# Attention output and x kept by channel: diagonal term on TensorE, three scans a round, later products turned, flag counted in round 4

## The chip, the cores and the metric

The kernel runs on one core of a Trainium2 chip. The core has TensorE (PE, matmuls; PEld is its weight load), VectorE (DVE), ScalarE (ACT), GpSimd (POOL) and SyncE (SP, which here issues the DMAs), each with its own instruction stream, joined by semaphores. The metric is the device time in microseconds; smaller is better. The kernel before has a median of 393.24 us over 3 runs (393.06 to 395.09). "Columns" below are the elements of a matmul's moving operand in the free dimension. An f32 matmul is recorded as two records (two passes); a matmul of operands marked fp32r is one record.

## The reference, cut to what matters

Three stages follow each other on a batch of 2, 768 tokens and 384 channels (8 heads of 48).

```python
# 1 attention with a decaying state, per head
for t in range(S):
    cur = einsum('bhd,bhe->bhde', u[None] * kt, vt)          # the diagonal term: only token t itself
    y[:, :, t] = einsum('bhd,bhde->bhe', rt, state + cur)
    state = wt[:, :, :, None] * state + einsum('bhd,bhe->bhde', kt, vt)
x = y by (batch, token, head*48)
# 2 gated block
h = gelu(x @ w_in);  u, v = halves of h (512 each);  v_n = (v - mean)/sqrt(var + 1e-6) * g_ln
v_s = einsum('ts,bsd->btd', w_sg, v_n) + b_sg;        x = x + (u * v_s) @ w_out
# 3 mixer
h = relu(x.T @ w_tok1) @ w_tok2;  u = x + h.T;        out = u + relu(u @ w_ch1) @ w_ch2
```

## The kernel before, in words

**Attention** runs in 12 chunks ("rounds") of 128 tokens, six per batch; chunk n is round n. The 8 heads lie in 4 pairs; a pair takes 112 partitions (48, 16 unused, 48). With w inside the chunk turned into running products, backward (`suf`, L886) and forward (`pre`, L897), k and r are scaled (`kp`, `rp`), so that one round is made of these products on TensorE: the scores kp x rp (`scores`, L1132), k turned to tokens by channels (`turn_kp`, L1140), the new state (`state_products`, L1159), and the output (`outputs`: the carried state times rp, L1178, plus the masked scores times v, L1182). The output has tokens on the partitions. The diagonal term r*u*k summed over a head's channels is made beside it: GpSimd multiplies r by k (L560) and by u (L568), VectorE sums over 48 channels (L919), GpSimd multiplies by v (L595), VectorE adds it to the output (L947).

The order on each engine is written out by hand. VectorE, in a round: two masks of the scores (L926), forward scans of the next chunk (a reciprocal and 4 scans of 127), the diagonal's sum, the output's sum, backward scans two chunks ahead (4 scans of 128), the state (L939). GpSimd: scale k of chunk n+1 (L578), r*k*u, scale r of chunk n+1 (L587), diagonal times v. In rounds 0 to 4 TensorE has a few matmuls on the identity as filler (L1272).

**A flag.** The scaling only holds for w in a range. ScalarE counts violations in ten pieces (`check_range`, L750, L752), TensorE sums them over the partitions (L1189), VectorE reduces the sum (`count_range`, L960 to L964), GpSimd loads it into a register, branches, and writes `flag` (L662). Work on x and on the later weights' low parts waits for the flag.

**The later products** have f32 accuracy by splitting each operand into a high part (fp32r) and the rest: every product is three matmuls (`three`, L1113 to L1115). High parts are copied by ScalarE (weights L820) or GpSimd, low parts are subtracted by GpSimd (weights L549) or VectorE. Weights pass through three landing buffers (`raw`). x lies by token; it is turned to channels by TensorE transposes before the first product of each stage ("xT", "uT", L1218). Jobs are named by kind, batch and index: v and u are the halves of x @ w_in, sg the token product, out, tok1, tok2, ch1, ch2. `SLOT` puts the first jobs between the parts of rounds 5 to 11 (three slots a round), `TAIL` lists the rest. A sg job is 18 matmuls of 384 columns, a u job 9 of 384, a v job 9 of 512.

Of the kernel before, what the change touches and what calls it, by code (L numbers as in the profile page):

```python
# [17 lines left out]
C = H * D  # L18
# [19 lines left out]
WR, KR, VR = 2, 2, 3  # L38
YR = 5
BR = 3  # L40
# [14 lines left out]
PIECES = ([("w_in", 2), ("w_in", 3), ("w_in", 0), ("w_in", 1)] + [("w_sg", i) for i in range(6)]  # L55
# [15 lines left out]
}  # L71
TAIL = ([("sg", 0, i) for i in range(3, 8)] + [("xT", 1, i) for i in range(6)] + [("out", 0, i) for i in range(6)]
        + [("v", 1, i) for i in range(6)] + [("u", 1, i) for i in range(8)] + [("sg", 1, i) for i in range(8)]
        + [("tok1", 0, i) for i in range(2)] + [("out", 1, i) for i in range(6)] + [("tok2", 0, i) for i in range(6)]
        + [("tok1", 1, i) for i in range(2)] + [("uT", 0, i) for i in range(6)] + [("tok2", 1, i) for i in range(6)]
        + [("ch1", 0, i) for i in range(NCF)] + [("uT", 1, i) for i in range(6)] + [("ch2", 0, i) for i in range(BT)]
        + [("ch1", 1, i) for i in range(NCF)] + [("ch2", 1, i) for i in range(BT)]
        + [("ch1", 2, i) for i in range(NCF)] + [("ch2", 2, i) for i in range(BT)])
# [3 lines left out]
OUT_BY = {"xT": "AD", "v": "A", "u": "A", "sg": "D", "out": "D", "tok1": "AD", "tok2": "D",  # L82
          "uT": "AD", "ch1": "AD", "ch2": "D"}
# [30 lines left out]
def build(nc, r, k, v, w, u, w_in, g_ln, w_sg, b_sg, w_out, tok1, tok2, ch1, ch2, w_turned, kr_turned, kr_rows, v_rows,  # L114
# [3 lines left out]
    y_slow = nc.dram_tensor("y_slow", (B * H, S, D), F32, kind="Internal").ap()  # L118
# [16 lines left out]
    x = at("x", XN, [PART, B, NC, C])  # L135
# [7 lines left out]
    wz = at("wz", Z + NC * FH, [PART, NC, NP, PART])  # L143
# [19 lines left out]
    wn = put("wn", [PART, WR, NP, PART])  # L163
    kr = put("kr", [PART, KR, 2, C])
    suf = put("suf", [PART, 2, NP, PART + 1])
    vn = put("vn", [PART, VR, C])
    pre = put("pre", [PART, NP, PART])
    kp = put("kp", [PART, NP, PART])
# [5 lines left out]
    yt = put("yt", [PART, BR, C])  # L174
    ub = put("ub", [PART, C])
    cmask = put("cmask", [PART, PART])
    ones = put("ones", [PART, PART])
    dg = put("dg", [PART, 2, H])
# [20 lines left out]
    krT = put("krT", [PART, KR, 2, NP, PART])  # L199
    u_row = at("u_row", Z + NC * FH - C, [1, C])  # L200
    rku = put("rku", [PART, 2, C])
# [5 lines left out]
    gy = put("gy", [PART, STEP, EW])  # L207
# [7 lines left out]
    with ExitStack() as ctx:  # L215
# [3 lines left out]
        def sem(name):  # L219
            return ctx.enter_context(nc.semaphore(name))  # L220

        w_in_, kr_in, krT_in, v_in = ([sem(f"{n}_in{i}") for i in range(ring)]
                                      for n, ring in (("w", WR), ("kr", KR), ("krT", KR), ("v", VR)))
# [3 lines left out]
        ub_in, gln_in, bsg_in = sem("ub_in"), sem("gln_in"), sem("bsg_in")  # L227
        ident_made, u_in, u_spread = sem("ident_made"), sem("u_in"), sem("u_spread")
# [7 lines left out]
        rp_done, rk_done, rku_done, base_done, flagged = (sem("rp_done"), sem("rk_done"), sem("rku_done"),  # L236
                                                          sem("base_done"), sem("flagged"))
# [8 lines left out]
        w_hi, w_hi_act, w_split, x1_hi, x1_split, stored = (sem("w_hi"), sem("w_hi_act"), sem("w_split"), sem("x1_hi"), sem("x1_split"),  # L246
                                                  sem("stored"))

        def u2T_place(g):

            half, g = divmod(g, 2 * BT)
            return u2T[half], slice(PART * g, PART * g + PART)
# [23 lines left out]
        def w_tile(n):  # L276
            return wz[:, n, :, :] if n < NC else wn[:, n % WR, :, :]
# [43 lines left out]
        steps, b1, b2, bs, by = ps[0][:, 0:PART], ps[1], ps[2], ps[3:5], ps[5]  # L321
        bc = ps[7][:, 0:CHECKS]

        def y_bank(n):
            return ps[6] if n < YR and n % 2 else by

# [19 lines left out]
        def _(sp):  # L346
            def load_w(n):
                if n >= NC + WR:
                    sp.wait_ge(pre_done, NP * (n - WR + 1))
                sp.dma_start(w_tile(n)[0:QP], w_turned[n]).then_inc(wz_in[n] if n < NC else w_in_[n % WR], 16)  # L350

            def load_krT(n):
                if n >= KR:
                    sp.wait_ge(kp_done, n - KR + 1)
                    sp.wait_ge(rp_done, n - KR + 1)
                sp.dma_start(krT[0:QP, n % KR], kr_turned[n]).then_inc(krT_in[n % KR], 16)

            def load_kr(n):
# [948 lines left out]


CONSTS = 1
V_CONSTS = 8  # L1310


# [30 lines left out]
```

## Time and profile before

| | |
|---|---|
| median of 3 runs | 393.24 us (393.06 to 395.09) |
| span of the profiled execution | 389.83 us |
| PE busy / PEld busy | 379.3 us (97%) / 354.8 us (91%) |
| DVE, ACT, POOL busy | 178.7 us, 105.3 us, 178.2 us |
| DMA | 30.69 MB, 79 GB/s on average |
| chain that ended last | PE 96%, issue 1%, DVE 1%, POOL 1% |

The span is that of one profiled execution, taken on the device from the first to the last instruction of the program; its own run time is not listed, and the median lies 3.4 us above the span. TensorE is the bound from the first microseconds. A busy PE is not PE at its peak: the clock that the throttle granted has its own line in slices of the span. VectorE and GpSimd are busy mostly in the first 110 us, that is, in attention.

### The profile page before, as it was taken

How to read it: one execution, taken by the hardware profiler on the slowest of the kernel's cores; microseconds unless marked ns; L12 is line 12 of the kernel's file. 1: busy time of each engine (PE TensorE's matmuls, PEld its weight loads, DVE VectorE, ACT ScalarE, POOL GpSimd, SP SyncE). 2: the span in 40 equal slices, each digit the busy share in tenths (PEclk: the TensorE clock that was granted, in tenths of full speed). 3: DMA queues.
4: the chain of work that ended last, by engine and by line, in shares of the span. 5: the costliest groups of instructions: out<-in, count | busy, mean ns of one | idle time of the engine just before them, and what ended most of it. 6: DMA issues, size and time to landing. Idle time of an engine off the chain costs nothing.

```text
span 389.8 us, 6178 instructions
## 1 busy us (share of the span) xinstructions
PE 379.3 (97%) x2380; PEld 354.8 (91%) x2380; DVE 178.7 (46%) x365; ACT 105.3 (27%) x193; POOL 178.2 (46%) x188
## 2 busy tenths in 40 slices
PE   8999699998999999999999999999999999999996
PEld 7899688897999998999999998889998899988996
DVE  6898788877644533224435753342113310133101
ACT  4457255664110204760012031340002300033000
POOL 4898889999556543966999920000000000000000
PEclk9999589998999999999999999999999999999999
DMA  8999947662102020020214300000010000100001
GB/s 237 284 290 290 251 145 215 206 214 77 66 0 83 0 83 0 2 80 2 82 41 141 102 4 0 2 0 22 20 40 2 0 21 21 40 2 0 22 20 40
DMA packets 15985, 30.69 MB, mean 79 GB/s; under 512 B 2002, under 2 KB 9555, under 8 KB 15955
## 3 DMA queue, kind: packets, MB, share of 16 engines
q1 hardware_dynamic: 15954, 30.29, 25.9%
q8 instruction: 19, 0.31, 0.4%
q14 instruction: 12, 0.09, 0.1%
HBM read 27.92 MB, written 2.36 MB: 78 GB/s over the span
## 4 chain that ended last, share of the span: by engine, by line
PE 96%; issue 1%; DVE 1%; POOL 1%; POOLq 0%; DVEq 0%
PE bank L1113 26%; PE bank L1114 26%; PE bank L1115 26%; PE bank L1182 5%; PE bank L1132 3%; PE bank L1178 3%; PE bank L1218 2%; PE bank L1272 2%; PE bank L1159 1%; PE bank L1140 1%; PE bank L1279 0%; DVE pre L897 0%; DVE dg L919 0%; POOL rku L568 0%; PE bank L1146 0%
## 5 line engine op out<-in xcount | busy, mean ns | idle before, releaser
L786 ACT ACTIVATE ha_hi<-bank 128x512 fp32r<-128x512 f32 x36 | 21.6, 599 | 107.7 <-PE bank L1115 107.7
L1021 DVE SCALAR_TENSOR_TENSOR ha_lo<-bank,ha_hi 128x512 fp32r<-128x512 f32 x36 | 24.9, 692 | 51.0 <-ACT ha_hi L786 51.0
L1113 PE MATMUL bank<-c_hi,ha_lo 128*128 128x384 f32 x144 | 48.2, 335 | 0.0
L1115 PE MATMUL bank<-c_hi,ha_hi 128*128 128x384 f32 x144 | 48.2, 334 | 0.0
L1114 PE MATMUL bank<-c_lo,ha_hi 128*128 128x384 f32 x144 | 48.2, 334 | 0.0
L1115 PE MATMUL bank<-u2T_hi,c_hi 128*128 128x512 f32 x108 | 42.1, 390 | 0.0
L1114 PE MATMUL bank<-u2T_lo,c_hi 128*128 128x512 f32 x108 | 42.1, 390 | 0.0
L1113 PE MATMUL bank<-u2T_hi,c_lo 128*128 128x512 f32 x108 | 42.0, 389 | 0.0
L1030 DVE TENSOR_TENSOR x<-bank,x 128x384 f32<-128x384 f32 (+1 forms) x12 | 6.5, 540 | 59.4 <-PE bank L1115 59.4
L1113 PE MATMUL bank<-sg_hi,z_lo 128*128 128x384 f32 x96 | 32.4, 337 | 0.0
L1114 PE MATMUL bank<-sg_lo,z_hi 128*128 128x384 f32 x96 | 32.1, 334 | 0.0
L1115 PE MATMUL bank<-sg_hi,z_hi 128*128 128x384 f32 x96 | 32.1, 334 | 0.0
L1182 PE MATMUL bank<-vn,am 128*128 128x48 f32 x192 | 28.3, 277 | 0.0
L1114 PEld LDWEIGHTS bank<-c_lo,ha_hi 128*128 128x128 f32 x144 | 27.0, 188 | 0.1
L1113 PEld LDWEIGHTS bank<-c_hi,ha_lo 128*128 128x128 f32 x144 | 27.0, 188 | 0.1
L1115 PEld LDWEIGHTS bank<-c_hi,ha_hi 128*128 128x128 f32 x144 | 27.0, 188 | 0.0
L1182 PEld LDWEIGHTS bank<-vn,am 128*128 128x128 f32 x192 | 26.6, 203 | 0.1
L1115 PEld LDWEIGHTS bank<-u2T_hi,c_hi 128*128 128x128 f32 x108 | 20.3, 188 | 4.2
L1113 PEld LDWEIGHTS bank<-u2T_hi,c_lo 128*128 128x128 f32 x108 | 20.3, 188 | 4.2
L1114 PEld LDWEIGHTS bank<-u2T_lo,c_hi 128*128 128x128 f32 x108 | 20.3, 188 | 4.1
L549 POOL TENSOR_TENSOR c_lo<-raw,c_hi 128x768 fp32r<-128x768 f32 x12 | 23.4, 1949 | 1.0
L1005 DVE SCALAR_TENSOR_TENSOR tmp<-bank,gln,bsg 128x384 f32<-128x384 f32 x16 | 9.9, 618 | 26.2 <-PE bank L1115 26.2
(138 smaller groups left out, 859.0 us busy)
## 6 DMA issues: line engine op xcount, KB each, us to landing
krT<-in_kr_turned SPq DMA_DIRECT2D x12, 448.0 KB, 5.8
kr<-in_kr_rows SPq DMA_DIRECT2D x12, 384.0 KB, 6.0
raw<-in_moe_w_ch SPq DMA_DIRECT2D x12, 384.0 KB, 3.2
vn<-in_v_rows SPq DMA_DIRECT2D x12, 192.0 KB, 5.5
raw<-in_moe_w_sg SPq DMA_DIRECT2D x6, 384.0 KB, 4.4
out<-x SPq DMA_DIRECT2D x11, 192.0 KB, 1.9
raw<-in_moe_w_in SPq DMA_DIRECT2D x4, 384.0 KB, 8.4
raw<-in_moe_w_tok SPq DMA_DIRECT2D x4, 384.0 KB, 3.1
```

What stands on the lines that cost most here:

```text
L549: gp.tensor_tensor(lo, raw_view(piece, hi), hi.bitcast(F32), ALU.subtract).then_inc(w_split, 1)
L786: sc.activation(ha[0][:, i, :], bank[:, :], ACT.Relu).then_inc(act_out, 1)
L1005: ve.scalar_tensor_tensor(tmp[:, i % 2, :], bank[:, 0:HALF], gln[:, dt:dt + 1], bsg[:, at_], ALU.mult, ALU.add).then_inc(dve_out, 1)
L1021: ve.scalar_tensor_tensor(ha[1][:, i, :], bank[:, :], 0.0, ha[0][:, i, :].bitcast(F32), ALU.max, ALU.subtract).then_inc(dve_out, 1)
L1113: te.matmul(dst, left[1], right[0], start=first, stop=False)
L1114: te.matmul(dst, left[0], right[1], start=False, stop=False)
L1115: return te.matmul(dst, left[0], right[0], start=False, stop=last)
L1132: ins = te.matmul(bs[i][:, tile(p)], kp[q, p, :], rp[q, n % 2, p, :], start=True, stop=True)
L1178: te.matmul(yb[:, 2 * D * p:2 * D * (p + 1)], rp[0:QP, n % 2, p, :], sbd[0:QP, n % 2, p, :], start=True, stop=False)
L1182: ins = te.matmul(yb[:, tile(h, D)], am[:, h, :], vn[:, n % VR, tile(h, D)], start=not inner, stop=i == 1 or not inner)
L1218: ins = te.transpose(bank[:, tile(kc)], x[:, b, i, tile(kc)], ident[:, :])
L1272: te.matmul(bank[:, 0:PART], ident[:, :], ident[:, :], start=True, stop=True)
```

## The change

x, the attention output and the final output lie by channel (`xr`, channels on the partitions, all 1536 tokens in the free dimension); the host turns the output back, and hands v in both layouts (`v_both`: by token in pairs of heads, and by channel). r and k by token are no longer loaded.

- Attention's output: the products have v and the state as weights of 32 columns, the scores and rp (128 columns) stream, four groups of 32 output partitions in turn. The diagonal is sum over d of u*r*k: GpSimd makes r*k on the turned tiles, TensorE multiplies by a block matrix of u (12 matmuls, again in groups of 32), VectorE multiplies by v (`t1`) and adds.
- Scans: the four runs of a chunk lie in one row of 4 x 129 with a head element between. The backward scan is two of 258, the forward one of 516 that goes over the heads, whose element is the reciprocal.
- `kp` has two buffers, the ring of turned k and r three.
- The first products need no transposes: ScalarE copies the high part of x (`xt_high`), GpSimd subtracts the low (`xt_low`). out, tok2 and ch2 swap weights and moving operand, so that they give channels by tokens; ch2 is 9 jobs of 36 matmuls of 512 columns in place of 12 of 36 of 384. Before tok1, x is turned to tokens ("x1t", 12 jobs of 3 transposes). In place of "uT", `u2_high` (ScalarE) and `u2_low` (VectorE) split x.
- The flag is counted in round 4 on VectorE, and TensorE sums the checks before that round's outputs; check 8 is moved from round 4 to round 3. GpSimd subtracts one piece of w_in before it waits for the count.
- Slots and tail: u jobs come first, sg starts in the first slot of round 10, and four sg jobs lie in the slots.

```diff
-    (5, 0): [("xT", 0, 0), ("xT", 0, 1)], (5, 1): [("xT", 0, 2), ("v", 0, 0)], (5, 2): [("xT", 0, 3)],
...
-    (9, 0): [("u", 0, 1)], (9, 1): [("u", 0, 3)],
-    (10, 0): [("u", 0, 5)], (10, 1): [("u", 0, 7)], (10, 2): [("sg", 0, 0)],
-    (11, 0): [("sg", 0, 1)], (11, 1): [("sg", 0, 2)],
+    (5, 0): [("u", 0, 0)], (5, 1): [("u", 0, 2)], (5, 2): [("v", 0, 0)],
+    (6, 0): [("v", 0, 1)], (6, 1): [("v", 0, 2)],
+    (7, 0): [("v", 0, 3)], (7, 1): [("v", 0, 4)], (7, 2): [("u", 0, 4)],
+    (8, 0): [("v", 0, 5)], (8, 1): [("u", 0, 6)], (8, 2): [("u", 0, 1)],
+    (9, 0): [("u", 0, 3)], (9, 1): [("u", 0, 5)], (9, 2): [("u", 0, 7)],
+    (10, 0): [("sg", 0, 0)], (10, 1): [("sg", 0, 1)],
+    (11, 0): [("sg", 0, 2)], (11, 1): [("sg", 0, 3)],
...
# VectorE: scans, diagonal, output
-                for p in range(NP):
-                    ve.tensor_tensor_scan(suf[0:QP, n % 2, p, 0:PART][:, ::-1], w_tile(n)[0:QP, p, :][:, ::-1],
-                                          steps[0:QP, :], 1.0, ALU.mult, ALU.bypass).then_inc(suf_done, 1)
+                for e in (slice(RUN // 2, RUN), slice(0, RUN // 2)):
+                    ve.tensor_tensor_scan(suf[0:QP, n % 2, e][:, ::-1], w_tile(n)[0:QP, e][:, ::-1], heads[:, ::-1], 1.0,
+                                          ALU.mult, ALU.add).then_inc(suf_done, 1)
...
-                for p in range(NP):
-                    ve.tensor_tensor_scan(pre[0:QP, p, 1:PART], w_tile(n)[0:QP, p, 0:PART - 1], steps[0:QP, 1:PART],
-                                          pre[0:QP, p, 0:1], ALU.mult, ALU.bypass).then_inc(pre_done, 1)
+                ve.tensor_tensor_scan(pre[0:QP, 0:RUN], w_tile(n)[0:QP, :], heads[:, 0:1].to_broadcast([QP, RUN]), 1.0,
+                                      ALU.mult, ALU.bypass).then_inc(pre_done, 1)
...
-                ve.tensor_reduce(dg[:, n % 2, :], rku[:, n % 2].rearrange("p (h d) -> p h d", h=H), AX.X, ALU.add).then_inc(dg_done, 1)
+                ve.tensor_tensor(t1[:, n % 2, :], b2[:, 0:C], vn[:, n % VR, VW:VW + C], ALU.mult).then_inc(t1_done, 1)
...
# GpSimd, rounds 1 to 4
             for n in range(1, YR):
                 scale_k(n + 1)
-                rku_products(n)
                 scale_r(n + 1)
-                if n == 1:
-                    diagonal_v(0)
-                diagonal_v(n)
                 rk_products(n + 1)
-            rku_products(YR)
+                if n > 1:
+                    xt_low(n - 2)
+            split_low("w_in", 0)
             pool.wait_ge(ok_counted, 1)
...
# TensorE
+            def diagonal(n):
+                pe.wait_ge(rk_done, n + 1)
+                pe.wait_ge(kn_copied, states(n))
...
+                for a in range(KC):
+                    for g in range(4):
+                        p, j = divmod(4 * a + g, 3)
+                        ins = te.matmul(b2[32 * g:32 * g + 32, tile(a)], ubd[0:QP, p, 32 * j:32 * j + 32],
+                                        rk[0:QP, n % 2, p, :], start=True, stop=True)
+                ins.then_inc(dg_done, 1)
...
-                outputs(n)
+                diagonal(n)
                 if n == YR - 1:
                     sum_range()
+                outputs(n)
...
# TensorE, output products: 16 new and (in all but chunks 0 and 6) 12 with the state, four groups in turn
+                for turn in itertools.zip_longest(*[parts(g) for g in range(4)]):
+                    for g, part in enumerate(turn):
+                        if part:
+                            a, left, right, first, last = part
+                            ins = te.matmul(yb[32 * g:32 * g + 32, tile(a)], left, right, start=first, stop=last)
...
-                        ins = three(bank[:, 0:C], cut(ha, ft, tile(i)), cut(c2, ft), ft == 0, ft == NCF - 1)
+                        ins = three(bank[:, :], cut(c2, ft, tile(i)), cut(ha, ft), ft == 0, ft == NCF - 1)
```

**TensorE's outputs of round 1.** In the kernel before, behind the state products (`vn,kn`), the carried state (`sbd`) and the masked scores (`am`) alternate, once per pair of heads:

```order
L1159 MATMUL bank<-vn,kn 48x48
L1178 MATMUL bank<-sbd,rp 128x96
L1182 MATMUL bank<-vn,am 128x48 x2
L1178 MATMUL bank<-sbd,rp 128x96
L1182 MATMUL bank<-vn,am 128x48 x2
```

In the changed kernel, at the same place, the diagonal (`rk,ubd`) comes first:

```order
L1173 MATMUL bank<-vn,kn 48x48
L1223 MATMUL bank<-rk,ubd 32x128 x12
L1209 MATMUL bank<-rp,sbd 32x128 x4
L1209 MATMUL bank<-am,vn 32x128 x4
L1209 MATMUL bank<-rp,sbd 32x128
L1209 MATMUL bank<-am,vn 32x128
```

12 matmuls (24 records) have become 40 (80 records), each on 32 columns of the array and with 128 streamed columns.

**GpSimd from the scaling of chunk 5 to the flag.** Before:

```order
L578 TENSOR_TENSOR kp<-krT,suf 112x512
L568 TENSOR_TENSOR rku<-rku,ub 128x384
L587 TENSOR_TENSOR rp<-krT,pre 112x512
L595 TENSOR_TENSOR yt<-vn,dg 128x384
L560 TENSOR_TENSOR rku<-kr 128x384
L568 TENSOR_TENSOR rku<-rku,ub 128x384
L707 TENSOR_LOAD oki
L708 COMPARE_AND_BRANCH
L662 COPY flag<-nhalf 128x1
```

Changed (`rk` is r*k, `xT_lo` the low part of x of chunk 2, `win_lo` that of w_in's first piece):

```order
L590 TENSOR_TENSOR kp<-krT_106,suf 112x512
L599 TENSOR_TENSOR rp<-krT_106,pre 112x512
L580 TENSOR_TENSOR rk<-krT_106 112x512
L606 TENSOR_TENSOR xT_lo<-xr,xT_hi 128x3x128
L569 TENSOR_TENSOR win_lo<-raw,win_hi 128x3x256
L715 TENSOR_LOAD oki
L716 COMPARE_AND_BRANCH
L670 COPY flag<-nhalf 128x1
```

Between the scaling of r and the load of the count lie three operations as before, but other ones.

**TensorE in round 10, after the scores.** Before, a u job (`xT,win`) follows the transposes:

```order
L1132 MATMUL bank<-rp,kp 128x128 x8
L1140 MATMUL bank<-ident,kp 128x112 x4
L1113 MATMUL bank<-xT_hi,win_lo 128x384
L1114 MATMUL bank<-xT_lo,win_hi 128x384
L1115 MATMUL bank<-xT_hi,win_hi 128x384
```

Changed, it is the first sg job, which waits for the last piece of w_sg to be split:

```order
L1145 MATMUL bank<-rp,kp 128x128 x8
L1154 MATMUL bank<-ident,kp 128x112 x4
L1126 MATMUL bank<-sg_hi,z_lo 128x384
L1127 MATMUL bank<-sg_lo,z_hi 128x384
L1128 MATMUL bank<-sg_hi,z_hi 128x384
```

On ScalarE and GpSimd the split of that piece (`sg_hi`, `sg_lo`) stands where it stood: after ScalarE's copy of round 10's turned k, and first on GpSimd in round 10.

## Rows read from the trace of the kernel before

**Rows 1.** Page, 40 equal slices of the span: granted clock of TensorE.
```profile
PEclk9999589998999999999999999999999999999999
```

**Rows 2.** Timeline of PE, rounds 3 to 5: start, duration, engine, line, operation.
```profile
25.61 1.16 PE L1132 MATMUL bank<-rp,kp 48*128 48x128 f32 x16
...
28.01 0.67 PE L1159 MATMUL bank<-vn,kn 128*64 128x48 f32 x16
28.75 0.43 PE L1178 MATMUL bank<-sbd,rp 112*128 112x96 f32 x2
...
31.53 1.16 PE L1132 MATMUL bank<-rp,kp 48*128 48x128 f32 x16
...
37.64 1.16 PE L1132 MATMUL bank<-rp,kp 48*128 48x128 f32 x16
42.01 1.51 PE L1218 MATMUL bank<-ident,x 128*128 128x128 f32 x6 [3.21 <-POOL flag L662]
```

**Rows 3.** Windows: stretch, length, busy by engine (instructions), granted clock, DMA.
```profile
40.68:50.91 10.23, 8.90 (x38) 8.54 (x39) 8.35 (x20) 2.27 (x4) 9.14 (x8) 0.50 0.92 260
...
95.29:98.70 3.41, 3.41 (x15) 3.41 (x13) 3.38 (x8) 1.36 (x2) 3.41 (x4) 0.50 0.38 115
```

**Rows 4.** Timeline of DVE, round 2 and the count.
```profile
20.91 1.29 DVE L926 TENSOR_TENSOR am<-bank,cmask 128x512 f32<-128x512 f32 x2
...
22.32 1.59 DVE L897 TENSOR_TENSOR_SCAN pre<-wz,pre,bank 112x127 f32<-112x127 f32 x4
...
25.10 1.35 DVE L886 TENSOR_TENSOR_SCAN suf<-wz,bank 112x128 f32<-112x128 f32 x4
...
40.85 0.15 DVE L964 CAST oki<-ok 128x1 int32<-128x1 f32 x1
```

**Rows 5.** Timeline of POOL, rounds 0, 2 and the flag.
```profile
10.06 1.18 POOL L578 TENSOR_TENSOR kp<-krT,suf 112x512 f32<-112x512 f32 x1 [3.28 <-PE bank L1140]
...
24.09 1.28 POOL L587 TENSOR_TENSOR rp<-krT,pre 112x512 f32<-112x512 f32 x1
...
41.69 0.18 POOL L662 COPY flag<-nhalf 128x1 f32<-128x1 f32 x1 [1.73 <-DVE oki L964]
```

**Rows 6.** Groups by line and shape, POOL: count, busy us, mean ns, idle before.
```profile
L560 POOL TENSOR_TENSOR rku<-kr 128x384 f32<-128x384 f32 x12 | 12.0, 1003 | 0.0
L595 POOL TENSOR_TENSOR yt<-vn,dg 128x384 f32<-128x384 f32 x12 | 9.9, 830 | 0.4 <-issue 0.4
```

**Rows 7.** Timeline of ACT, the last check.
```profile
35.82 1.26 ACT L750 ACTIVATE junk<-check_w,ok 128x1152 bf16<-128x1152 f32 x1
```

**Rows 8.** Timeline of POOL and PE, end of round 9.
```profile
92.55 1.27 POOL L587 TENSOR_TENSOR rp<-krT,pre 112x512 f32<-112x512 f32 x1
...
93.92 1.16 PE L1132 MATMUL bank<-rp,kp 48*128 48x128 f32 x16 [1.62 <-issue]
```

**Rows 9.** Timeline of ACT and POOL, round 10.
```profile
95.84 0.53 ACT L724 COPY kn<-bank 128x448 f32<-128x448 f32 x1 [1.84 <-PE bank L1140]
96.39 0.83 ACT L820 CAST sg_hi<-raw 128x768 fp32r<-128x768 f32 x1
...
97.58 1.82 POOL L549 TENSOR_TENSOR sg_lo<-raw,sg_hi 128x768 fp32r<-128x768 f32 x1
```

**Rows 10.** Timeline of PE, tail: transposes of batch 1, ch1 and ch2 matmuls.
```profile
132.60 2.13 PE L1218 MATMUL bank<-ident,x 128*128 128x128 f32 x18
...
337.23 0.39 PE L1113 MATMUL bank<-u2T_hi,c_lo 128*128 128x512 f32 x1
...
340.89 0.39 PE L1114 MATMUL bank<-u2T_lo,c_hi 128*128 128x512 f32 x1
...
382.05 0.34 PE L1113 MATMUL bank<-c_hi,ha_lo 128*128 128x384 f32 x1
...
386.56 0.34 PE L1115 MATMUL bank<-c_hi,ha_hi 128*128 128x384 f32 x1
```

More of the change, by code:

```diff
@@ L52 @@
 SLOW_OPS = 12
-PIECES = ([("w_in", 2), ("w_in", 3), ("w_in", 0), ("w_in", 1)] + [("w_sg", i) for i in range(6)]
+PIECES = ([("w_in", 0), ("w_in", 2), ("w_in", 3), ("w_in", 1)] + [("w_sg", i) for i in range(6)]
           + [("w_out", i) for i in range(2)] + [("tok1", i) for i in range(2)] + [("tok2", i) for i in range(2)]
@@ L111, in states, with u2_parts, u2_count, build @@
     return (NC - 1) * (n // NC) + min(n % NC + 1, NC - 1)
-def build(nc, r, k, v, w, u, w_in, g_ln, w_sg, b_sg, w_out, tok1, tok2, ch1, ch2, w_turned, kr_turned, kr_rows, v_rows,
+def u2_parts(b, i):
+    g, end = S * b + HALF * (i // 3), S * b + HALF * (i // 3) + HALF
+    cuts = [g] + [c for c in range(2 * WIDE, B * S, 2 * WIDE) if g < c < end] + [end]
+    return list(zip(cuts, cuts[1:]))
+def u2_count(b, i):
+    return sum(len(u2_parts(e, j)) for e in range(b + 1) for j in range(6 if e < b else i + 1))
+def build(nc, r, k, v, w, u, w_in, g_ln, w_sg, b_sg, w_out, tok1, tok2, ch1, ch2, w_turned, kr_turned, v_both, u_turned,
           out):
@@ L245, in build, with u2T_place @@
         gated, g_hi, g_split = sem("gated"), sem("g_hi"), sem("g_split")
[L246 to L252, printed above, removed]
+        w_hi, w_hi_act, w_split, stored = sem("w_hi"), sem("w_hi_act"), sem("w_split"), sem("stored")
+        def u2T_place(m, start, end):
+            half, start, end = start // (2 * WIDE), start % (2 * WIDE), (end - 1) % (2 * WIDE) + 1
+            return [e[:, m, start:end] for e in u2T[half]]
         def u2T_block(b):
@@ L628, in split_gated @@
                                  ).then_inc(g_split, 1)
-            low = {5: [("w_in", 0)], 6: [("w_in", 1), ("w_sg", 0)], 7: [("w_sg", 1)], 8: [("w_sg", 2), ("w_sg", 3)],
+            low = {6: [("w_in", 1), ("w_sg", 0)], 7: [("w_sg", 1)], 8: [("w_sg", 2), ("w_sg", 3)],
                    9: [("w_sg", 4)]}
@@ L853, in _ @@
                     take_state(n)
+                if n == YR:
+                    xt_high(n - 2)
+                    xt_high(n - 1)
                 for job in slot_jobs(n, 2):
                     take_job(*job)
+            for tc in range(NC):
+                xt_high(NC + tc)
             for kind, b, i in TAIL:
@@ L862, in _ @@
                     normal(1, NC - 1)
-                if (kind, b, i) == ("u", 1, 7):
-                    for tc in range(NC):
-                        x1_high(0, tc)
-                if kind == "out" and b:
-                    x1_high(1, i)
+                if kind == "tok2":
+                    u2_high(b, i)
         @block.vector
@@ L1097, in _ @@
                     stats(b, i)
-                if (kind, b, i) == ("u", 1, 7):
-                    for tc in range(NC):
-                        x1_low(0, tc)
-                if kind == "out" and b and i:
-                    x1_low(1, i - 1)
-                if (kind, b, i) == ("out", 1, NC - 1):
-                    x1_low(1, i)
+                if kind == "tok2" and i:
+                    u2_low(b, i - 1)
+                if kind == "tok2" and i == 5:
+                    u2_low(b, i)
         @block.tensor
```

462 lines of the change are left out of this document (239 added, 223 removed), and 3 rows, old and new, of the table SLOT.

## The prediction, on record before the result

> **What bounds the kernel now.** I read the page's slices and the chain of waits first. The reader is to see there that TensorE is busy 97% of the span and is 96% of the chain: what counts is TensorE's work, its few waits, and its clock. The clock line [rows 1] is full except in two places, near 41 to 51 us and near 95 us. The timeline of TensorE then shows why. A round of attention is 5.92 us from scores to scores (25.61 to 31.53), and hardly a gap lies in it; behind the scores of round 5 (37.64, 1.16 us long) TensorE waits 3.21 us for the flag [rows 2], and the clock is at 0.50, 1.2 GHz, for 10.2 us [rows 3]. At 92.3 it waits 1.62 us for the scaled r of round 10, which GpSimd ends at 93.82 [rows 8]; the clock is then at 0.50 for 3.41 us, fully busy [rows 3]. From there to the end TensorE is never idle: what the tail saves is work alone. The timelines of the other engines [rows 4 to 7] give the prices.
>
> **The span and the median.** The sum is made against the profiled span, 389.8 us; the median, 393.24, is 3.4 above it, and I take the same distance for the changed kernel.
>
> **Output and diagonal on TensorE, each round.** Before, the outputs of a round take from 28.75 to the next scores at 31.53, 2.7 us [rows 2]: 24 records. Now there are 28 matmuls for the output and 12 for the diagonal, 80 records of 128 columns. A record of 128 columns takes 0.11 us at full clock (18 transposes in 2.13 us [rows 10]), so 80 one after the other would be 8.9 us. They are not one after the other if groups of the array work side by side. The scores do that: 16 records of 128 columns, alternating between two halves of the array's rows, take 1.16 us and not 1.8 [rows 2]. For groups of columns the nearest row is the state product, two groups (64 and 48 columns): 16 records in 0.67 us, 0.6 without the last one's way out, 0.037 each [rows 2]; since a record's weights of 128 columns alone cost 0.11 us elsewhere, two groups of about half that, in turn, would give 0.05 each or 0.8 us. So groups of columns overlap too. Four groups are not shown. If they overlap as the scores' two do, a round is 7 + 3 turns of 2 records each, 20 x 0.112 = 2.24, and some 0.2 for the two starts: 2.45. The bounds are 2.45 and, with nothing side by side, 8.9; at the state product's 0.037 for each record it is 2.95; in pairs only, 4.5. I take 2.45, the rate of the scores: they too stream 128 columns a record, while the state product's 48 are too short to hide its weights. That is 0.25 less per round, in 10 rounds; in chunks 0 and 6, which have no carried state, 56 records give 1.77 against 1.8, nothing.
>
> The Trainium skill, "TensorE: Matmul & The Clock Gate", in "Measured speedup vs the span model", gives four groups a gain of 3.07 and not 4. No run here shows four. By that page the 80 records would take about 2.9 us and the change would lose about 5.5 us of the gain below; this is the same size as the third rival's, which is worked out from the state product.
>
> **Rounds 0 to 3.** VectorE's four backward scans take 1.35 us, the four forward ones 1.59 [rows 4]. The columns stay the same (516 for 512), so what goes is the fixed part of the scans saved. From 1.35 for 4, the last of them with its own end, I take 1.25 for two of 258 and 1.2 for one of 516; the bounds of the forward one are 1.6 (nothing fixed) and 0.4 (all fixed, which a scan's work by element excludes). In round 0, where TensorE waits for the scaled operands, both lie on the path: 0.1 + 0.4 before the first scores, 0.4 again between mask and scaled r of chunk 1; the 3.28 us for which GpSimd waited to scale k [rows 5] lies beside it. Gain 0.9. In rounds 1 to 3 two loops bind at nearly the same length. TensorE: what lies from the scores to the outputs stays, 25.61 to 28.75 [rows 2] less a pause of 0.1 behind the state products, 3.0, and 2.45 for diagonal and outputs: 5.45. The loop of data: scores 1.2, masks 1.29, reciprocal and scan 1.4, GpSimd's scaling of r 1.28 [rows 4, 5], and hand-overs: 5.35. VectorE is filled to 5.15: 1.25 + 1.4 + 0.5 (the diagonal's multiply, costed as the sum over it that it replaces) + 0.5 + 1.2 + 0.3. GpSimd drops two multiplications of 0.83 and 1.0 [rows 6] and gets one low part of x (costed at 1.0, as a subtraction of that size): no bound. 5.92 to 5.45, three times: gain 1.4.
>
> **The flag.** VectorE's count no longer ends last (before, 41.0 [rows 4]); what is late next is GpSimd. From the scores of round 4: masks end at 2.5, the scan at 3.9, r is scaled at 5.35, then r*k (112x512, as the scaling of k, 1.18 [rows 5]) to 6.5, the low part of x to 7.6 (ScalarE's high part is there at 6.5: scores and transposes 1.7, copies 0.53 for k [rows 9] and an estimated 0.75 for the state, last check 1.26 [rows 7] and its read-out to 4.4, two pieces of w_in at 0.83 [rows 9], x at 0.5), one low part of w_in (1.82 [rows 9]) to 9.4, then 0.7 from the count to the flag as before [rows 4, 5], and 0.15 to TensorE: 10.3. Before it was 31.53 to 42.01, 10.5 [rows 2]. Gain 0.2. Meanwhile TensorE stands behind the last check (at 4.4) with the outputs of round 4, so round 5's scores start 6.4 later and end at 7.6: it still waits 2.7 us for the flag. All of round 5 is queued behind.
>
> **The clock after it.** Before, 8.90 us of work ran at half clock [rows 3], a loss of 4.45. Now a u job, dense in columns, follows at once, before outputs on few columns. I take a loss of 2.8 (bounds: nothing, and 4.45): gain 1.65.
>
> **Rounds 5 to 11.** Output and diagonal, six rounds of 0.25: 1.5. The 18 transposes of batch 0 go: 2.0. GpSimd loses 1.65 per round in rounds 7 to 11, which is 3.3 in rounds 8 and 9 alone, against the 1.62 by which it was late for round 10's scores; a piece of w_in that it now subtracts before the flag is 1.8 more. The 1.62 us and the loss of half of 3.41 at half clock [rows 3, 8] go: gain 3.3.
>
> **A new wait.** In round 10 the sg job stands right behind the transposes. It needs the sixth piece of w_sg split. ScalarE copies its high part after the turned k (0.53, 0.83), GpSimd subtracts (1.82) [rows 9], all of it behind the same transposes: TensorE waits 0.1 + 1.4 + 0.1 + 1.8 = 3.4 us. In the kernel before, two u jobs, the outputs and the state products stood between these transposes and the first sg job, and covered this. Behind it are the diagonal, the outputs and VectorE's whole round. The clock will fall as it did for 1.62 us of waiting; I take 2.2 us lost (1.7 as in rows 3's second stretch, 4.45 as in its first). Cost 5.6.
>
> **Tail.** The fourth sg job moves from tail to slots, no change. 18 transposes go, 2.0; "uT" and "x1t" are 36 each. ch2: 432 matmuls at 0.1735 (26 steps from 382.05 to 386.56) are 74.9 us, 324 of 512 columns at 0.2288 (16 steps from 337.23 to 340.89) are 74.1 [rows 10]: 0.8. The last add and store are a third wider, 0.1. Gain 2.7. The splits of x are behind other jobs: the first low parts have four sg jobs (12.5 us) as cover, the last tok2 of batch 0 has two tok1 jobs (6.2 us).
>
> **Sum:** 0.9 + 1.4 + 0.2 + 1.65 + 1.5 + 2.0 + 3.3 - 5.6 + 2.7 = 8.05 us less: span 381.8, time 385.2.
>
> **Rivals.**
> First, the flag comes in time, as its count is a round's half earlier: for it, the count itself is ready at 5.5 us; against it, GpSimd's row of work. It would save 2.7 and 2.8 more: 379.7. Chance 0.10.
> Second, the wait for w_sg is hidden or harmless (GpSimd and ScalarE far enough ahead): for it, the piece is in SBUF by then; against it, ScalarE's place behind the transposes. 5.6 more: 379.6. Chance 0.07.
> Third, four groups take 0.037 us for each record: 0.5 a round in ten rounds and 0.3 in two, 5.6: 390.8. For it, the state product's rate; against it, that there the weights, 0.06 us for 64 columns, explain the rate. Chance 0.11.
> Fourth, slower: column groups run in pairs at most, one mechanism in every round's outputs and diagonal. 80 records at 0.056 are 4.5, 2.05 more in ten rounds, 1.4 in two: 23 more, 408. It decides from 0.042 us a record on, where it eats the 8 us. For it, only two groups are seen; against it, that the array's parts are alike. Chance 0.08.
> Fifth, the rounds do not get shorter, since VectorE, the loop of data and TensorE are within 0.3 us of each other and each waits a little for the next: 2 to 5 us more, 389. Chance 0.08.
> The forecast itself: 0.56.
>
> **How the numbers follow.** A difference of 0.5% (2 us) is what a measurement can tell here. Faster than 391.3: the forecast, rivals one and two, most of the fifth, a third of the third: 0.80. Within: the rest of the third and of the fifth: 0.10. Slower: 0.10. The range 379 to 391 takes in the first three cases and the fifth, and just the third.
>
> **What would show it.** In the profile after: outputs and diagonal in 2.4 to 2.5 us (or 3, or over 4); scores of round 5 near 35.8; TensorE released by the flag near 39.6 after 2.7 us; no wait before round 10's scores, but 3.4 us behind its transposes, released by the low part of w_sg; clock at 0.50 in two places; ch2 matmuls 0.229 apart. It is wrong if groups of 32 columns don't overlap, if a DMA (v by two layouts, 0.43 MB a chunk) comes late in the first rounds, or if VectorE's long scan is not near 1.2 us.

## The result: 399.0 us, slower by 1.5%

The changed kernel takes 399.0 us (median of 4 runs, 397.8 to 400.3) against 393.15 for the kernel before (4 runs, 391.2 to 395.1): ratio 1.015, interval 1.011 to 1.019. The forecast was 385.2 us, with a range from 379 to 391. Its profiled span is 398.7 us, before 389.8; the forecast span was 381.8. So 17 us have to be found. Single executions of some kernels below take over 1.5% longer than the fastest of the same kernel; the ratios leave these out, and where too few are left none is given.

The page first, three lines of it: slices of the span for the granted clock and for the DMA engines, and the chain of waits by engine.

```profile
PEclk9996997999889999999999999999999999999999
DMA  8998067636110202001112510000000000100001
PE 87%; DVE 6%; issue 3%; DMA 2%; SPq 1%; DVEq 0%
```

Against [rows 1] the clock now falls in four stretches (the windows below), and VectorE has 6% of the chain. The list of TensorE's waits (sum, times, longest) names the places:

```profile
PE bank L1145 <- DVE kp L928: 5.2, 2, 2.7
PE bank L1209 <- issue: 4.7, 3, 2.4
PE bank L1126 <- issue: 3.4, 1, 3.4
PE bank L1223 <- issue: 2.8, 2, 2.1
PE bank L1312 <- POOL ident L541: 1.8, 1, 1.8
PE bank L1126 <- POOL flag L670: 1.4, 1, 1.4
```

The third line is the wait for w_sg that the prediction priced, and the last is the flag's. The first, second and fourth are new to it; the fifth, at the start, is there in the kernel before too (1.8). From the windows view (stretch, length, PE, PEld, DVE, ACT, POOL busy, clock, DMA share, GB/s), the stretches at 1.2 GHz:

```profile
33.85:40.67 6.82, 6.60 (x63) 5.67 (x63) 2.60 (x4) 2.39 (x5) 2.41 (x3) 0.51 0.68 181
64.57:71.40 6.83, 6.25 (x29) 5.26 (x29) 6.59 (x15) 2.06 (x4) 3.48 (x6) 0.51 0.34 78
98.70:102.10 3.40, 3.40 (x65) 3.02 (x58) 1.96 (x4) 1.81 (x4) 3.31 (x3) 0.51 0.02 5
112.35:115.80 3.45, 3.45 (x12) 3.45 (x12) 0.00 (x0) 0.00 (x0) 1.60 (x2) 0.52 0.35 115
```

20.5 us at half clock, against 13.6 before [rows 3]; each stretch begins in or just behind one of the waits that are new against the kernel before.

**First new wait: the scaled k.** VectorE's timeline in round 6 (start, duration), then GpSimd's at the same time:

```profile
57.05 1.23 DVE L919 TENSOR_TENSOR_SCAN pre<-wn,bank 112x516 f32<-112x516 f32 x1
58.20 6.90 DVE L928 TENSOR_TENSOR kp<-krT,suf 112x512 f32<-112x512 f32 x1
65.02 0.55 DVE L943 TENSOR_TENSOR t<-bank,vn 128x384 f32<-128x384 f32 x1
```
```profile
57.60 1.29 POOL L580 TENSOR_TENSOR rk<-krT 112x512 f32<-112x512 f32 x1
58.84 1.01 POOL L606 TENSOR_TENSOR xT_lo<-xr,xT_hi 128x384 fp32r<-128x384 f32 x1
59.81 1.19 POOL L599 TENSOR_TENSOR rp<-krT,pre 112x512 f32<-112x512 f32 x1
60.97 1.82 POOL L569 TENSOR_TENSOR win_lo<-raw,win_hi 128x768 fp32r<-128x768 f32 x1
62.75 1.80 POOL L569 TENSOR_TENSOR sg_lo<-raw,sg_hi 128x768 fp32r<-128x768 f32 x1
64.51 1.71 POOL L621 TENSOR_TENSOR z_lo<-vf,z_hi 128x512 fp32r<-128x512 f32 x1
```

Scaling k (two operands and the result in SBUF) takes 0.67 and 0.68 us in rounds 5 and 9, 1.78 in round 10, and 6.90 here; it ends 0.6 us after the start of the last operation of GpSimd's unbroken row, and that last one takes 1.71 where others of its kind take 1.26 to 1.29. Rounds 7 and 8 are alike (5.40 and 7.14 us, ending 0.59 us after the start of a z_lo). TensorE waits for it ahead of the scores of rounds 7 and 9; the third line below is the diagonal of round 9, late because the state was late:

```profile
65.15 2.08 PE L1145 MATMUL bank<-rp,kp 48*128 48x128 f32 x16 [2.75 <-DVE kp L928]
...
92.67 1.16 PE L1145 MATMUL bank<-rp,kp 48*128 48x128 f32 x16 [2.43 <-DVE kp L928]
...
98.03 1.03 PE L1223 MATMUL bank<-rk,ubd 112*32 112x128 f32 x24 [2.06 <-issue]
```

**Second: pauses inside the outputs.** In rounds 1 to 3 TensorE stops in the middle of 56 records that no semaphore separates:

```profile
19.00 0.31 PE L1209 MATMUL bank<-am,vn 128*32 128x128 f32 x4 [1.12 <-issue]
...
25.95 0.30 PE L1209 MATMUL bank<-am,vn 128*32 128x128 f32 x2 [1.22 <-issue]
...
34.07 0.42 PE L1209 MATMUL bank<-am,vn 128*32 128x128 f32 x1 [2.39 <-issue]
```

219, 344 and 469 records of TensorE's matmuls stand ahead of them: they are 125 apart. The page's row for the instruction queue has more packets than before (19 then, 0.31 MB), each 16 KB:

```profile
q8 instruction: 23, 0.38, 0.4%
```

Such packets start at 16.43, 23.36 and 31.31 us and take 1.1 to 1.3; TensorE goes on 1.4 to 1.5 us after each has ended. I call what such a packet brings an instruction block; that one block holds 125 of the records is read from the distance of the pauses.

### The profile page after: what moved, and what is told of

It is laid out like the page before. It is cut to its first block, busy times and chain, and to the rows that moved or that the text cites. A ratio compares the mean times of both kernels' runs of the same rounds, so it can differ in the third digit from the quotient of the medians.

```text
span 398.7 us, 7096 instructions
## 1 busy us (share of the span) xinstructions
PE 374.7 (94%) x2874; PEld 332.1 (83%) x2874; DVE 182.3 (46%) x295; ACT 106.2 (27%) x197; POOL 170.9 (43%) x175
## 3 DMA queue, kind: packets, MB, share of 16 engines
HBM read 25.98 MB, written 2.36 MB: 71 GB/s over the span
## 4 chain that ended last, share of the span: by engine, by line
PE 87%; DVE 6%; issue 3%; DMA 2%; SPq 1%; DVEq 0%
PE bank L1126 25%; PE bank L1127 24%; PE bank L1128 24%; DVE kp L928 5%; PE bank L1209 4%; PE bank L1145 3%; PE bank L1223 2%; DMA vn<-in_v_both 2%; PE bank L1154 1%; PE bank L1173 1%; PE bank L1254 1%; PE bank L1312 1%; PE bank L1160 0%; DVE suf L909 0%; SPq L374 0%
## 5 line engine op out<-in xcount | busy, mean ns | idle before, releaser
L1126 PE MATMUL bank<-ha_hi,c_lo 128*128 128x512 f32 x108 | 42.0, 389 | 0.0
L1127 PE MATMUL bank<-ha_lo,c_hi 128*128 128x512 f32 x108 | 42.0, 389 | 0.0
L1128 PE MATMUL bank<-ha_hi,c_hi 128*128 128x512 f32 x108 | 42.0, 389 | 0.0
L1126 PE MATMUL bank<-sg_hi,z_lo 128*128 128x384 f32 x96 | 33.3, 347 | 3.4 <-issue 3.4
L1053 DVE TENSOR_TENSOR xr<-bank,xr 128x512 f32<-128x512 f32 (+1 forms) x9 | 6.0, 661 | 57.9 <-PE bank L1128 57.9
L1209 PE MATMUL bank<-am,vn 128*32 128x128 f32 x384 | 20.2, 290 | 4.7 <-issue 4.7
L1126 PEld LDWEIGHTS bank<-ha_hi,c_lo 128*128 128x128 f32 x108 | 20.3, 188 | 4.2
L1128 PEld LDWEIGHTS bank<-ha_hi,c_hi 128*128 128x128 f32 x108 | 20.3, 188 | 4.2
L1127 PEld LDWEIGHTS bank<-ha_lo,c_hi 128*128 128x128 f32 x108 | 20.3, 188 | 4.1
L928 DVE TENSOR_TENSOR kp<-krT,suf 112x512 f32<-112x512 f32 x6 | 22.6, 3761 | 0.0
```

The lines of the kernel that those rows point to most:

```text
L928: ve.tensor_tensor(kp[0:QP, n % 2], krT[n % KR][0:QP, 0], runs(suf[:, n % 2, :], 2), ALU.mult).then_inc(kp_done, 1)
L1053: ve.tensor_tensor(dst[:, done:WIDE], bank[:, done:WIDE], dst[:, done:WIDE], ALU.add).then_inc(dve_out, 1)
L1126: te.matmul(dst, left[1], right[0], start=first, stop=False)
L1127: te.matmul(dst, left[0], right[1], start=False, stop=False)
L1128: return te.matmul(dst, left[0], right[0], start=False, stop=last)
L1209: ins = te.matmul(yb[32 * g:32 * g + 32, tile(a)], left, right, start=first, stop=last)
```

## The experiments

Theory A: VectorE's operation with both operands in SBUF cannot get through while GpSimd's operations follow each other without a break. Theory D, later H: the pauses are instruction blocks that come late. Each edit below is made on the changed kernel. The runs were on several chips, on which the kernel before took 391.1 to 393.2 us, so ratios to it compare better than times do.

**A wait for VectorE ahead of GpSimd's row**

```
                 if YR < n < NCH - 1:
                     scale_r(n + 1)
+                    pool.wait_ge(kp_done, n + 2)
                 for piece in low.get(n, []):
```

> The changed kernel with one wait more on GpSimd: after it has scaled r of the next round it waits until VectorE has scaled k of the same round, and only then takes its row of low halves. Theory A (VectorE's scaling of k, with both operands and the result in SBUF, cannot get through while GpSimd runs its row of SBUF operations back to back): the three operations of 6.90, 5.40 and 7.14 us fall to at most 1.6 us each; TensorE's waits for them of 2.75 (65.2) and 2.43 us (92.7) and the two waits that come of the late state (0.75 at 83.2, 2.06 at 98.0) go, 8.0 us, and with them most of the slow clock of 64.6 to 71.4 and 98.7 to 102.1, some 3 us; GpSimd's rows end up to 0.7 us later. 399.0 less 8 to 11: 388 to 391 us. Rival B (the operation is late for its own inputs, or long by its layout): it stays over 3 us and the time stays at 399 within 1. Rival C (the waits are covered by something that ends just as late, such as z_low for the later products): k's scaling is short and the time falls by less than 3 us.

Measured: 387.1 us (4 runs), ratio to the kernel before 0.987 (0.982 to 0.993); span 385.9, 12.8 less than the changed kernel (on another chip; by the two ratios it is 11 us). Scaling k, count, busy and mean ns, here, and (L928) in the changed kernel:

```profile
L929 DVE TENSOR_TENSOR kp<-krT,suf 112x512 f32<-112x512 f32 x6 | 6.9, 1154 | 0.0
```
```profile
L928 DVE TENSOR_TENSOR kp<-krT,suf 112x512 f32<-112x512 f32 x6 | 22.6, 3761 | 0.0
```

All four waits for it and for the late state are gone, and the time is below the 388 to 391 expected. One wait instruction turns 1.5% slower into 1.3% faster. Rivals B and C fall. The longest is 2.20, over my 1.6.

**Gaps alone**

```
+                    pool.wait_ge(rp_done, n + 2)        # behind scale_r(n + 1)
                 for piece in low.get(n, []):
                     split_low(*piece)
+                    split_count[0] += 1
+                    pool.wait_ge(w_split, split_count[0])
```

> The changed kernel with waits on GpSimd for its own operations only: after scaling r of the next round, and after each low half of a weight piece, it waits for that operation's own semaphore before it issues the next. Order and work are as they were; what is new is a short gap between GpSimd's operations. Theory A (the long operation of VectorE gets in at the first gap of GpSimd's row): the scaling of k ends within about 0.7 us of the end of r's scaling, so lasts about 2 to 2.4 us in place of 6.90, 5.40 and 7.14; time 388 to 392 us, as with the other wait. Rival B (VectorE gets a share of each of GpSimd's operations, and gaps do nothing): it lasts 5 to 7 us as before, 399 us within 1. Rival C (a gap of some tens of ns is too short, but the mechanism is the same): long here and short in the kernel whose GpSimd waits for VectorE.

Measured: 386.3 us, ratio 0.986 (0.983 to 0.990), mean of k's scaling 1198 ns. GpSimd waits for nobody here, only for the end of its own operation; between the scaled r and the next operation lie 0.08 us (62.50 to 62.58). That is enough, so it is the row without a wait in it that holds VectorE off, not any order of data. Where VectorE gets in is not as I said:

```profile
59.25 2.20 DVE L933 TENSOR_TENSOR kp<-krT,suf 112x512 f32<-112x512 f32 x1
```
```profile
60.85 1.65 POOL L599 TENSOR_TENSOR rp<-krT,pre 112x512 f32<-112x512 f32 x1
```

Round 6's operation ends at 61.45, 0.6 us after the start of the scaled r, which now takes 1.65 in place of 1.19, and over a microsecond before the pause. So VectorE does not use the pause itself; it goes in ahead of the operation behind which the new wait stands, and that one becomes 0.45 longer. With the first edit it gets in at the same place. In rounds 6 to 8 of the changed kernel it is ahead of the last of the row, in its round 10 ahead of one in the middle. What picks the place stays open.

**The stream shifted by 64 matmuls**

```
-            keep_busy(4, ps[6])
+            for e in range(68):
+                g = e % 4
+                te.matmul(ps[6][32 * g:32 * g + 32, 0:32], ident[:, 0:32], ident[:, 0:32], start=True, stop=True)
```

> The changed kernel with 64 more matmuls in TensorE's stream ahead of the first scores: the four 128-column matmuls on the identity there are replaced by 68 small ones of 32 columns, four groups side by side, about as long in sum. Nothing else is moved. Theory D (TensorE's three pauses inside the outputs of rounds 1 to 3, 1.12, 1.22 and 2.39 us with no semaphore behind them, are instruction blocks that come too late: they lie 125 records apart, and each ends about 1.3 us after a 16 KB transfer of the instruction queue): each block then begins 64 records earlier in the program, at the first state products of rounds 1 to 3, ahead of which TensorE waits 0.4 us anyway, so the pauses leave the outputs, and most of 4.7 us goes, with the clock's fall at 33.9 to 40.7 (about 3 us): 391 to 395 us. If a pause shows at all it is 61 to 67 records earlier in the stream. Rival E (the outputs themselves stall, by their operands, by the PSUM bank or by other DMA traffic at that time): the pauses stay at the 29th, 32nd and 35th record of the outputs, 399 us within 1.

Measured: 399.7 us, ratio 1.023 (1.015 to 1.030), the changed kernel's own. The expectation was worked out wrongly: a matmul of this data type leaves two records (28 make the 56 of the outputs), so the stream moved by 128 records, about a whole block, and the test could not tell. Only one thing spoke for D: a new pause of 1.27 us at record 221, the second of round 0's outputs, where there had been none.

**The last piece of w_sg in round 9**

```
-   9: [("w_sg", 4)], 10: [("w_sg", 5)],                       # ScalarE, high
+   late = {9: [("w_sg", 5)], NCH - 1: [("w_out", 0), ("w_out", 1)]}
-            first = {10: [("w_sg", 5)]}                       # GpSimd, low, ahead of round 10
+            after_z = {9: [("w_sg", 5)]}                      # behind round 9's z_low
```

> The changed kernel with the high half of the last piece of w_sg copied by ScalarE in round 9, after the normalisation, in place of round 10 after k's copy, and its low half made by GpSimd at the end of round 9 in place of the beginning of round 10. Theory F (TensorE's wait of 3.41 us behind round 10's transposes is for this piece alone, and with the slow clock of 112.4 to 115.8 it costs 5 us): the first gate product starts at about 107.9 in place of 111.2, 393.5 to 396 us. Rival G (the next input, GpSimd's last low half of z, or a later wait for GpSimd or VectorE takes it back): less than 1.5 us, 397.5 to 399.5.

Measured: 392.6 us, but from 384.2 to 394.1, so no verdict on its own; k's scaling still took up to 7.15 us in it. Its trace does show the place: the first sg matmul follows round 10's transposes without a wait (105.81 and 106.18).

**Both edits**

> The changed kernel with two earlier edits at once: GpSimd waits for VectorE's scaled k before its row of low halves, and the last piece of w_sg is split in round 9. If the two gains are apart (theory F of the wait behind round 10's transposes), the time is that of the first edit alone, 387.1, less 3.4 to 5.6 us: 381.5 to 384 us. Rival G (z's last low half or k's copy is next there): 386 to 388 us.

Measured: 383.8 us (382.6 to 386.3), ratio 0.980 (0.975 to 0.986), 3.3 under the first edit alone (387.1, another chip), its span 4.8 under; the intervals of the two ratios overlap, so the second edit's own gain is not apart from nothing by the runs. The wait behind round 10's transposes is 1.77 us, not nothing:

```profile
95.20 0.41 PE L1126 MATMUL bank<-sg_hi,z_lo 128*128 128x384 f32 x1 [1.77 <-issue]
```

GpSimd's row now ends with that low half at 95.11, behind z's at 93.3: what is next is GpSimd's own work. But the clock is full in all 40 slices of the page, in this execution; in the other three its mean is 0.982 to 0.995:

```profile
PEclk9999999999999999999999999999999999999999
```

By the traces theory F holds for the place, and G for part of the size. What is left in this kernel is the second finding: 5.3 us of pauses at records 219, 344 and 469.

**Half a block, with both edits**

```
-            keep_busy(4, ps[6])
+            keep_busy(2, ps[6])
+            for e in range(34):                               # the same small matmuls
```

> As the kernel with both edits, and 32 more matmuls ahead of the first scores, 64 records of the trace, half a block (two of the 128-column matmuls there are replaced by 34 small ones). Theory H: the pauses stay 125 records apart and come 64 records earlier in the program: in round 1 to 3 at the 5th to the 12th of the 16 records of the state products, not in the outputs. Since a block is asked for 125 records ahead and takes about 7 us to come while a round of 122 records needs 5.5, the rounds stay as long as the blocks take, so no more than 1.5 us is gained. Rival E (the outputs stall by themselves): the pauses stay inside the outputs at their 29th to 35th record, time unchanged too; where the pauses lie tells the two apart, not the time.

Measured: 384.5 us (382.0 to 387.9), no change, as H has it. The pauses are at records 220, 345 and 470, practically where they were, and these are now in the state products:

```profile
18.11 0.47 PE L1173 MATMUL bank<-vn,kn 128*48 128x48 f32 x10 [1.33 <-issue]
...
33.51 0.29 PE L1173 MATMUL bank<-vn,kn 128*64 128x48 f32 x4 [2.30 <-issue]
```

They belong to a place in the stream, not to the outputs. Rival E falls.

**The pieces of w_in later, with both edits**

```
-            load_raw(0)    # and 1, 2, ahead of the loop, issued at 15.5 to 23 us
+                if n == 5: # behind load_krT(7): 33 us.  The middle place: n == 4, behind load_w(7): 28 us
+                    for i in range(SLOTS):
+                        load_raw(i)
```

> As the kernel with both edits, and the first three pieces of w_in (1.15 MB, three transfers issued at 15.7 to 21 us) are issued after k and r of round 7, at about 33 us. Theory H (the instruction blocks are asked for when TensorE enters the block before, and wait 3.0 to 5.5 us among data transfers, because all 16 DMA engines are busy until 37 us; in an idle stretch the same wait is 0.25 us): the blocks of rounds 2 and 3 start at most 2.5 us after TensorE enters the block before; the second and the third pause inside the outputs (1.22 and 2.39 us) fall to under 0.5 us together, and the first (1.12) stays or shrinks; 2.5 to 3.5 us faster than the kernel with both edits, and up to 3 more of clock, unless the pieces of w_in now land too late for round 5. Rival I (the pauses have to do with TensorE's stream alone, not with traffic): pauses as before, no gain.

Measured: the third pause (2.39 us) is gone altogether; its block was asked for no later than 27.4, when TensorE entered the block before, and started at 29.55, 2.1 us later in place of 5.3. The first two stay, 1.72 and 1.49: while they lasted, other loads filled the DMA engines as before, so for these two it is not shown that the traffic delays the block. Round 4's scores start at 33.53, not 35.49. Then w_in is late: TensorE waits 5.5 us for the flag. 387.7 us in all, so as a kernel it is worse, and the expectation of less than 0.5 us for both later pauses held for one.

> As the kernel with both edits (383.8), and the three pieces of w_in are issued after w of round 7 (about 28 us), between the place that the changed kernel has (15.5 to 23 us) and the late one (33 us). Theory H (instruction blocks wait among data transfers): the third block, asked for at 26.6, no longer waits 5.4 us for its start (24.2 to 32.0 in the kernel with both edits lie such waits), but under 3.5, so the third pause of 2.39 us falls under 0.8; the pieces land by 37 us, and the first product no longer waits 5.5 us for the flag as with the late place, but about 2. 2 to 3.5 us faster: 380.5 to 382 us. Rival I (the late place helped the third pause by chance): pauses of 1.4, 1.5 and 2.4 us as before and 383.8 within 1.

Measured: the third pause is gone again, the block starts 1.3 us after TensorE has entered the block before (26.33, 27.65), and the wait at the first product is 2.1. Scores of round 5 start at 39.04 in place of 41.80. The time, 384.5 us from 379.8 to 386.4, where 380.5 to 382 was expected, does not show it; the four runs spread by more than the gain.

**Fewer records, with both edits**

```
+                        m = 64 if g % 2 == 0 and j < 2 else 0 if g % 2 and j else 32
-                        ins = te.matmul(b2[32 * g:32 * g + 32, tile(a)], ubd[0:QP, p, 32 * j:32 * j + 32],
+                        ins = te.matmul(b2[32 * g:32 * g + m, tile(a)], ubd[0:QP, p, 32 * j:32 * j + m],
```

> As the kernel with both edits, and in the diagonal and in the state's share of the outputs two neighbouring groups of 32 columns of one pair of heads become one of 64: 8 matmuls in place of 12 each, so a round has 106 records in place of 122 (the outputs are also ordered by tile of 128 channels). Theory H: a block lasts 125/106 of a round, so the three pauses of 4.7 us shrink by about 0.9 us a round, 2 to 3 us in sum, and the time falls by 2 to 4 us. Rival J (order by tile breaks the running side by side of four groups): the outputs take over 1.8 us in place of 1.57, and the time is the same or up to 2 us worse.

Measured: 395.1 us, ratio 1.008 (1.005 to 1.011), 11 us more than the kernel with both edits on the same chip, where 2 to 4 less were expected. There are no pauses inside the rounds any more, but since a round now takes 7.3 us this says little. Of the diagonal's 16 records 15 start from 16.97 on, and the first of the outputs at 18.36:

```profile
16.97 1.71 PE L1223 MATMUL bank<-rk,ubd 112*64 112x128 f32 x15
...
18.36 0.32 PE L1206 MATMUL bank<-rp,sbd 112*64 112x128 f32 x1
```

0.09 us a record, where 24 records of 32 columns need 0.68 us, 0.028 each. A group of 64 and one of 32 columns in turn do not run side by side: two neighbours of the same width start 0.01 us apart (17.64, 17.65), and at each change of width the next starts 0.20 later (17.10, 17.30; 17.44, 17.64). The diagonal has no accumulation and kept its order, so it is the width. The outputs take 3.0 us to the next scores (18.36 to 21.37), over rival J's 1.8; both width and order changed in them, so what the order costs is not shown.

**Round 5's first product behind the outputs, and all together**

```
-    (5, 0): [("u", 0, 0)], (5, 1): [("u", 0, 2)],
+    (5, 1): [("u", 0, 0), ("u", 0, 2)],
```

> As the kernel with both edits, and round 5's first product is issued behind the outputs instead of ahead of the diagonal, so that TensorE's wait for GpSimd's flag (2.07 us at 43.0) lies beside 2.3 us of diagonal and outputs. If nothing else waits for the flag on the way, 2 us faster: 381.5 to 382.5. Rival K (x of round 0 of the second kind, VectorE's x_tile, waits for the flag too, and the outputs of round 6 for it; or round 5's products shift everything behind by the same): 383.8 within 1.

Measured: 383.0 us (381.7 to 384.6), where 381.5 to 382.5 was expected; TensorE's wait in round 5 falls from 2.1 to 1.2 us and is now ahead of the outputs, where VectorE's addition for round 4 ends last. So it is rival K in another form, and 0.8 us less than the kernel with both edits is within the spread, and the two were on different chips.

> Both of the two edits just named, on the kernel with both earlier edits. If they are apart: 383.8 less 4 to 5.5 us, 378.5 to 380 us; if the earlier end of round 4 only makes the wait for the flag longer (GpSimd's row ahead of the flag is bound by the landing of w_in and by ScalarE's copies of it), it is no better than the better of the two.

Measured: 382.3 us (378.5 to 385.2), ratio 0.980 (0.975 to 0.984), span 377.0, the shortest of all; 378.5 to 380 was expected. It is not apart from the kernel with both edits by its runs; by its trace TensorE's pauses in the outputs are 2.1 us in place of 5.3.

## Why the prediction was wrong, step by step

- **Output and diagonal on TensorE: right.** 24 records of the diagonal take 0.68 us and 56 of the outputs 1.68 to the next scores, 2.36 against 2.45 forecast:

```profile
40.80 0.86 PE L1223 MATMUL bank<-rk,ubd 112*32 112x128 f32 x24
...
41.59 0.39 PE L1230 MATMUL bank<-ok,ones 128*128 128x10 f32 x2
...
43.59 1.16 PE L1145 MATMUL bank<-rp,kp 48*128 48x128 f32 x16
```

  Against [rows 2], where the 24 records of the outputs alone took 2.7. The third and fourth rival are out: 0.028 us a record beside the 0.11 of one alone [rows 10] is four times. The gain of 3.07 that the prediction took from the Trainium skill, "TensorE: Matmul & The Clock Gate", section "Measured speedup vs the span model", is the page's for four groups of the array's rows at 512 columns; carrying it over to groups of columns was a step of mine. It is not borne out for these columns, which in a long stream gain four.
- **Rounds 0 to 3: half right.** The scans are as priced (1.26 for two of 258, 1.23 for one of 516), and the first scores came at 7.84. But "a round is 5.45" left out what TensorE reads its program from. A round went from 66 records to 122, and a block is 125; while the DMA engines are full a block takes 7 us from TensorE's entry into the one before (19.00 to 25.95; 25.95 to 34.07 is 8.1). So a round cannot be much shorter than the block's way: 6.84 and 6.75 us between scores, then 8.76 for the third, 22.4 for the three where the forecast had 16.4. In them lie 4.7 us of pauses, and the clock is at half from 33.85 on, around the end of the longest. That the pauses belong to a place in the stream is shown by the half-block shift, and that traffic delays the block for the third alone.
- **The flag: right in kind.** TensorE waited 1.4 us for it (2.7 forecast; 3.2 before [rows 2]), though the scores of round 5 came at 43.6, not 35.8. The clock stayed full behind it; the half clock came earlier, behind the third pause.
- **Rounds 5 to 11: this step failed most.** It said that GpSimd, 1.65 us a round shorter, is no longer late for round 10's scores, a gain of 3.3 (1.62 of waiting and 1.7 of clock), and put VectorE's scaling of k at nothing. What GpSimd lost were also its gaps: in rounds 6 to 8 it now did its work without a break, and the scaling of k came to 5.4 to 7.1 us. TensorE waited 8.0 us for it and for the late state. Undone, it is worth 12.8 us of span (11 by the ratios), about two thirds to three quarters of the 17. The gain itself came: in the three kernels without these waits nothing is late before round 10's scores, for which TensorE waited 1.62 [rows 8]. The sign had been in the trace of before, in round 10, where k's scaling takes four times its usual length beside three GpSimd operations in a row, and I did not read it:

```profile
98.03 2.87 DVE L905 TENSOR_TENSOR kp<-krT,suf 112x512 f32<-112x512 f32 x1
```

  The Trainium skill states the ground for this in "SBUF — State Buffer", section "SBUF: two separate sides": VectorE and GpSimd have one pair of ports in common, held exclusively for a whole instruction, and a VectorE operation with two SBUF inputs takes part in it. The trace agrees that one of them stands still while the other works. By that page the wait would end with GpSimd's current operation, at most 1.8 us here; measured, it lasts over the ends of five in round 6, and over two with either edit.
- **The new wait: right.** 3.41 us against 3.4 forecast, at the place forecast. Behind it lie 3.45 us at half clock, 1.7 lost where the forecast took 2.2:

```profile
111.21 0.41 PE L1126 MATMUL bank<-sg_hi,z_lo 128*128 128x384 f32 x1 [3.41 <-issue]
```

- **The tail: right.** It is without a gap as before. From the last record of the outputs to the end it takes 269.8 us, before 276.1; 3.1 of that is the sg job that moved into the slots, and 3.2 are left against 2.7 forecast.

The sum, as an estimate from these rows: 8.0 us of waits for k and the state, 4.7 of pauses, and 9.9 lost to the half clock (half of TensorE's 19.7 busy us in the four stretches) where 5.0 were forecast, less 1.3 for the flag, are 16.3 of the 17. None of the rivals was this. Slower had its chance of 0.10 mostly from groups of columns that run in pairs, and these ran as forecast; the fifth, rounds that do not get shorter, has the right sign for rounds 1 to 3, for another reason.

With GpSimd's row broken and w_sg early, the kernel takes 383.8 us, near the forecast 385.2. That is luck in part: its trace has 5.3 us of pauses that the forecast did not know, no loss of clock where the forecast had 5.0, and 1.77 us of its wait for w_sg in place of 3.4.

## What to carry to other kernels

Work taken off an engine is a gain only if nobody lived in its gaps: before GpSimd's row is closed up, list VectorE's operations that have all operands in SBUF and see what they take beside an unbroken stretch. Count instructions too when matmuls are cut small; here a loop of 122 records a turn, near the 125 of a block, took as long as its blocks took to come, 6.8 to 8.8 us while the DMA engines were full. An operation with one long instance among short ones in the trace of before is a warning, even where it costs nothing.

## What the hardware showed unexpectedly

- GpSimd's unbroken row stretched VectorE operations of 0.67 us to 5.40, 6.90 and 7.14. A wait for its own end behind one operation of the row, a pause of 0.08 us, cut the 6.90 to 2.20; VectorE got in ahead of that operation, not in the pause.
- An instruction block of TensorE starts 1.3 to 5.4 us after TensorE enters the block before while other transfers fill the DMA engines, and 0.25 us after (42.93, 43.18) when they are idle.
- Four groups of 32 columns: 0.028 us a record of 128 columns. Groups of 64 and 32 in turn: 0.09, with 0.20 us at each change of width.
